# An attention, DFT and FFN kernel on one core: ScalarE's table load started early by a constant copy, filling work of PE as wide products, and the rounding of batch 1's y moved ahead of batch 0's last statistics

## Chip, cores and metric

The kernel runs on one core of one Trainium2 chip, as one launch. The metric is the device time in microseconds (us); the comparison is between medians of executions of the two kernels.

The engines are called PE (TensorE), DVE (VectorE), ACT (ScalarE), POOL (GpSimd) and SP (SyncE, which here only starts transfers). PEld are PE's weight loads.

## The reference, cut to what matters

```python
# attention: 2 batches, 8 heads, 768 rows, head width 64, all float32
mask = q_bucket[:, :, :, None] == k_bucket[:, :, None, :]   # buckets: signs of q @ proj and k @ proj, 6 bits
scores = np.where(mask, scale * q @ k.T, -1e9)
x = softmax(scores) @ v                    # -> (2, 768, 512)
# mixing and feed-forward
mixed = np.real(np.fft.fft(np.fft.fft(x, axis=1), axis=2))
u = x + mixed
un = (u - mean(u)) / np.sqrt(var(u) + 1e-6)              # per row
x = u + np.maximum(un @ w_ch1, 0) @ w_ch2                # 512 -> 2048 -> 512
# gated output
gate = sigmoid(causal depthwise convolution of x, 5 taps)
out = (gate * (x @ w_val)) @ w_out
```

## The kernel before, in words

Every engine has its own instruction list, written out by hand and run in order; semaphores (`wait_ge`, `then_inc`) are the only ties between the lists. So what stands ahead in an engine's list holds back what is behind it. A wide float32 product is made of three products of rounded values: each operand is split into a `_hi` part (rounded by ACT) and a `_lo` part (the rest, by DVE or POOL).

**Start.** SP and ACT issue the loads of the first head (`q_raw`, `k_raw`), `proj` and others. POOL sets the constants: it adds 1 to `consts_ready` for `minus_scale`, `w_q`, `w_k`, `zero`, `minus_half` and `ident`, and once more when `ident` holds the unit matrix. ACT then waits for `k_raw` and casts it to `k_a` (`round_k`, L701), casts `q_a` (L705) and copies `q_b` (L710). POOL makes `k_b` (L497) and the low half of `q_a` (L502). PE in the meantime makes the hash bits of q and k (L1299), DVE turns them into bits (L1000), PE into bucket numbers (L1305), and DVE writes the other halves of `q_b` and `k_b` (L1004, L1005). The first scores (L1346) need all four operands. Between these steps PE does filling work: `keep_busy(n)` makes n transposes of the unit matrix into bank 7, three times (17, 5 and 14), and nobody reads them. ACT's first computing instruction is the one of L701, and a table load is placed in front of it.

**Attention.** Eight pairs of heads run through 12 slots each: scores, row minimum (DVE L1012), exponential (ACT L718), transposes (L1413), product with v (L1363).

**DFT.** For each batch b the rows are folded, and PE forms y, the DFT along the sequence, in five banks: `sequence_step(b, t, blocks)` (L1386) adds step t to some of the blocks 0 to 4, and `seq_full` tells that a block is complete. ACT rounds each block to `y_hi` (L840), DVE takes the rest `y_lo` (L1170), and both copy a mirrored edge of the blocks 0 to 2 (L843, L1174). PE then does the DFT along the features in four steps per batch (`feature_dft`, L1494). Step 0 waits block by block for `y_lo`, step 1 for all mirrored edges.

**Statistics.** Each batch has six tiles of 128 rows; tile n of 0 to 5 is batch 0. For each: the sine bank is copied (ACT L816, `sine_part`), DVE forms cosine minus and plus sine (`cos_and_sin`, L1126), POOL and DVE add them to x (L630, L633, `mirrored_add` L1136), DVE takes the moments (L1090), the aggregate (L1094) and the sum with eps (L1098), POOL the inverse root `rstd` (L618), DVE the `shift` (L1104), ACT writes the normalised tile `un` (`normalise`, L807), PE transposes it (`transpose_un`, L1468), ACT rounds it (`unT_hi`, L799) and DVE takes the rest (`unT_lo`, L1112).

The loops of the two batches overlap. Before the change the order around the turn from batch 0 to batch 1 is:

- ACT: normalise of tile 3; five rounds of y of batch 1; three mirror copies; `unT_hi` of tile 3; normalise of tiles 4 and 5; then sine copies, with `unT_hi` of tiles 4 and 5 between.
- DVE: statistics of tiles 4 and 5 with their shifts; five `y_lo` of batch 1; three mirror copies; `unT_lo` of tile 3; cosine step; `unT_lo` of tile 4; cosine step; and so on.
- PE: the last step of the sequence DFT of batch 1, transpose of tile 3, features step 0, transpose 4, step 1, transpose 5, steps 2 and 3.
- POOL: the inverse root of tile 5 stands ahead of the first add of batch 1.

**FFN and output.** After features step 3 PE begins the FFN of batch 0: `ffn1` (L1549) waits for the cosine step of tile group 2 of batch 1 and for `unT_lo` of tile 5; `open_acc` (L1535) for the last cosine step. From there on the lists are long loops over 16 blocks of the FFN for each batch (L1549, L1563), and then the value and output products.

Of the kernel before, what the change touches and what calls it, by code (L numbers as in the profile page):

```python
# [6 lines left out]
def attention_fft_ffn_gate_kernel(nc, qT, kT, v, proj, w_ch1, w_ch2, w_val, conv_wT, w_out,  # L7
# [19 lines left out]
    P = 128  # L27
# [24 lines left out]
    with ctx:  # L52
# [632 lines left out]
        def _(act):  # L685
# [4 lines left out]

            def scale_first(h):

                act.wait_ge(qk_loaded[h], loads(0, h))
                act.mul(q_raw[h][:, :], q_raw[h][:, :], -SCALE).then_inc(q_scaled, 1)
# [137 lines left out]

            for b in range(B):
                for blk in range(5):
                    act.wait_ge(seq_full, 5 * b + blk + 1)

                    need(act, feat_full, 4 * b)
                    src = PS[:, SEQ_BANKS[b][blk], :]
                    size = HALF + 1 if blk < 3 else HALF
                    act.copy(y_hi[:, blk, 0:size], src[:, 0:size]).then_inc(y_hi_done, 1)  # L840
                for blk in range(3):
                    act.wait_ge(y_hi_done, 8 * b + blk + 1)
                    act.copy(y_hi[:, blk, HALF + 1:HALF + P], y_hi[:, blk, 1:P].bitcast(F32)).then_inc(y_hi_done, 1)  # L843
                if b:
                    unT_hi(T - 3)
                    normalise(T - 2)
                    normalise(T - 1)
                for t in range(T):
                    n = b * T + t
                    if t in (0, 2, 3):  # L850
                        sine_part(4 * b + t)
                    if b and t < 2:
                        unT_hi(T - 2 + t)
                    if not b and t >= LAG:
                        unT_hi(n - LAG)
                    if 2 <= t < (T - 1 if b else T):
                        normalise(n - 2)
                    if b and t == 3:
                        relu(0, 0)
# [112 lines left out]
        def _(dve):  # L972
# [190 lines left out]
            dve.wait_ge(fold_edge, 12)  # L1163
            for b in range(B):
                for blk in range(5):

                    dve.wait_ge(y_hi_done, 8 * b + blk + 1)
                    size = HALF + 1 if blk < 3 else HALF
                    src = PS[:, SEQ_BANKS[b][blk], :]
                    dve.tensor_tensor(y_lo[:, blk, 0:size], src[:, 0:size], y_hi[:, blk, 0:size].bitcast(F32),  # L1170
                                      ALU.subtract).then_inc(y_lo_done, 1)
                for blk in range(3):
                    dve.wait_ge(y_lo_done, 8 * b + blk + 1)
                    dve.tensor_copy(y_lo[:, blk, HALF + 1:HALF + P], y_lo[:, blk, 1:P].bitcast(F32))\  # L1174
                       .then_inc(y_lo_done, 1)
                if b:
                    unT_lo(T - 3)
                for t in range(T):
# [3 lines left out]
                    if t % 2:  # L1182
                        mirrored_add(n)
                    if t >= 2:
# [4 lines left out]
                    if b and t < 2:  # L1189
                        unT_lo(T - 2 + t)  # L1190
# [6 lines left out]
                moments(n)  # L1197
                aggregate(n)
                shift(n - 1)
                add_eps(n)  # L1200
                shift(n)
# [90 lines left out]
        def _(pe):  # L1292
# [151 lines left out]
            keep_busy(14)  # L1444
# [60 lines left out]
            for b in range(B):  # L1505
                if b:
# [234 lines left out]
```

## Time and profile before

| | |
|---|---|
| median of 3 runs | 635.16 us (634.46 to 636.32) |
| the profiled execution | 635.57 us |
| its span, first to last instruction | 633.9 us |
| mean granted clock of PE | 0.997 |
| instructions | 11055 |
| PE busy | 618.7 us, 98% |
| DVE busy | 346.1 us, 55% |
| ACT busy | 317.4 us, 50% |
| POOL busy | 250.7 us, 40% |
| DMA, mean over the span | 66 GB/s |

All times below are in microseconds from the start of the span, unless marked ns. A row of a timeline gives the start, how long the group lasted from the start of its first to the end of its last instruction, the engine, the line of the kernel, the operation, what it writes and reads, and how many instructions are merged (x5). In brackets stands how long the engine had been idle before, and what ended that. Successive instructions of one engine overlap a little, so the step from start to start is shorter than one's own duration. The granted clock is a share of PE's full 2.4 GHz: 1.00, or 0.50 for 1.2 GHz.

### The profile page before, as it was taken

To read this page: it belongs to the slowest core of one execution; us is meant where nothing else is said; L and a number is where in the kernel's file an instruction comes from. 1 tells how busy PE (TensorE), PEld (TensorE's weight loads), DVE (VectorE), ACT (ScalarE), POOL (GpSimd) and SP (SyncE) were. 2 spreads that over 40 slices of the span, in tenths; PEclk is the share of its full clock that TensorE was granted. 3 is DMA by queue.
4 is the path that set the end of the run, shared out by engine and by line. 5 is a ranking of instruction groups with operands and counts; after the bars stand their busy time and mean duration, and the time that the engine had idled before them with its cause. 6 is when DMAs were issued, how large, how long until landed. Compare 5 with 4: busy or idle time off the path is not lost.

```text
span 633.9 us, 11055 instructions
## 1 busy us (share of the span) xinstructions
PE 618.7 (98%) x3766; PEld 505.4 (80%) x3766; DVE 346.1 (55%) x587; ACT 317.4 (50%) x609; POOL 250.7 (40%) x213
## 2 busy tenths in 40 slices
PE   5899999999999999989999999999999999999998
PEld 4676777767777676989888888888888888888786
DVE  2888888887888875787111111117333333349820
ACT  3777777777777883464333222225233332444242
POOL 4533444333347664346333233327444434403140
PEclk9999999999999999999999999999999999999999
DMA  5762323223333020000211222620222221000202
GB/s 133 193 151 71 88 63 88 73 76 87 80 103 90 12 64 1 1 1 23 79 48 53 66 66 66 199 68 13 87 66 66 66 66 49 1 1 2 83 18 99
DMA packets 34267, 42.15 MB, mean 66 GB/s; under 512 B 3520, under 2 KB 22208, under 8 KB 34240
## 3 DMA queue, kind: packets, MB, share of 16 engines
q1 hardware_dynamic: 32272, 37.38, 20.6%
q0 software_dynamic: 1728, 4.02, 2.6%
q10 hardware_dynamic: 240, 0.39, 0.3%
q8 instruction: 17, 0.28, 0.2%
q14 instruction: 10, 0.08, 0.0%
HBM read 38.63 MB, written 3.15 MB: 66 GB/s over the span
## 4 chain that ended last, share of the span: by engine, by line
PE 90%; DVE 4%; ACT 2%; issue 2%; POOL 1%; DMA 1%; ACTq 0%; POOLq 0%; DVEq 0%
PE banks L1563 21%; PE banks L1549 21%; PE banks L1346 12%; PE banks L1363 11%; PE banks L1413 10%; PE banks L1642 5%; PE banks L1386 2%; PE banks L1494 2%; PE banks L1626 2%; PE banks L1299 2%; DVE x_then_u_then_gate L1213 1%; DMA k_raw<-in_k 1%; PE banks L1421 1%; PE banks L1305 1%; PE banks L1468 1%
## 5 line engine op out<-in xcount | busy, mean ns | idle before, releaser
L1143 DVE SCALAR_TENSOR_TENSOR h_lo<-banks,h_hi 128x512 fp32r<-128x512 f32 x64 | 35.4, 558 | 169.4 <-ACT h_hi L831 169.4
L1012 DVE TENSOR_REDUCE row_min<-banks 128x1 f32<-128x768 f32 x96 | 91.7, 956 | 33.9 <-PE banks L1346 33.4
L718 ACT ACTIVATE prob<-banks,row_min 128x768 f32<-128x768 f32 x96 | 87.0, 906 | 31.3 <-DVE row_min L1012 31.2
L1549 PE MATMUL banks<-unT_hi,w_hi 128*128 128x512 f32 (+1 forms) x256 | 86.4, 338 | 0.2 <-DVE h_lo L1143 0.2
L1549 PE MATMUL banks<-unT_hi,w_lo 128*128 128x512 f32 (+1 forms) x256 | 86.3, 337 | 0.0
L1549 PE MATMUL banks<-unT_lo,w_hi 128*128 128x512 f32 (+1 forms) x256 | 86.2, 337 | 0.0
L1413 PE MATMUL banks<-ident,prob 128*128 128x128 f32 x576 | 79.3, 273 | 1.3 <-ACT probT L350 1.3
L563 POOL TENSOR_TENSOR w_lo<-w_stage,w_hi 128x512 fp32r<-128x512 f32 x32 | 45.3, 1414 | 86.6 <-ACT w_hi L749 86.6
L1413 PEld LDWEIGHTS banks<-ident,prob 128*128 128x128 f32 x576 | 68.1, 140 | 6.7 <-issue 1.8
L831 ACT ACTIVATE h_hi<-banks 128x512 fp32r<-128x512 f32 x64 | 31.2, 490 | 79.4 <-PE banks L1549 79.3
L1363 PE MATMUL banks<-probT,v_in 128*64 128x384 f32 x384 | 69.0, 494 | 0.0
L568 POOL TENSOR_TENSOR w_lo<-w_stage,w_hi 128x512 fp32r<-128x512 f32 x32 | 42.2, 1317 | 67.2 <-ACT w_hi L754 67.2
L1563 PE MATMUL banks<-h_lo,w_hi 128*128 128x512 f32 (+1 forms) x256 | 66.0, 339 | 0.0
L1563 PE MATMUL banks<-h_hi,w_hi 128*128 128x512 f32 (+1 forms) x256 | 66.0, 339 | 0.0
L1563 PE MATMUL banks<-h_hi,w_lo 128*128 128x512 f32 (+1 forms) x256 | 65.6, 338 | 0.0
L754 ACT CAST w_hi<-w_stage 128x512 fp32r<-128x512 f32 x32 | 19.9, 621 | 88.6 <-PE banks L1563 88.6
L1213 DVE SCALAR_TENSOR_TENSOR x_then_u_then_gate<-x2T,taps,x_then_u_then_gate 128x384 f32<-128x384 f32 (+1 forms) x64 | 58.9, 926 | 4.9 <-DVE x_then_u_then_gate L1213 2.6
L1346 PE MATMUL banks<-k_a,q_a 128*128 128x384 f32 x192 | 57.6, 381 | 3.8 <-POOL q_a L502 2.8
L350 ACT COPY probT<-banks 128x384 f32<-128x384 f32 x104 | 49.0, 479 | 22.4 <-PE banks L1413 22.1
L497 POOL TENSOR_TENSOR k_b<-k_raw,k_a 64x768 fp32r<-64x768 f32 x16 | 29.2, 1826 | 72.1 <-ACT k_a L701 72.0
L1346 PEld LDWEIGHTS banks<-k_a,q_a 128*128 128x128 f32 x192 | 30.0, 191 | 32.6 <-issue 29.7
L1549 PEld LDWEIGHTS banks<-unT_hi,w_hi 128*128 128x128 f32 x256 | 48.1, 188 | 7.3 <-DVE h_lo L1143 0.4
(156 smaller groups left out, 1191.0 us busy)
## 6 DMA issues: line engine op xcount, KB each, us to landing
w_stage<-in_moe_w_ch SPq DMA_DIRECT2D x64, 256.0 KB, 2.8
q_raw<-in_q SPq DMA_DIRECT2D x32, 192.0 KB, 3.3
k_raw<-in_k SPq DMA_DIRECT2D x30, 192.0 KB, 3.6
v_in<-in_v SPq DMA_DIRECT2D x16, 192.0 KB, 2.8
out<-y_out SPq DMA_DIRECT2D x12, 256.0 KB, 2.0
seq_tables_sb<-in_dft POOLq DMA_DIRECT2D x6, 386.0 KB, 3.5
wvo_stage<-in_moe_w_val SPq DMA_DIRECT2D x1, 1024.0 KB, 5.7
wvo_stage<-in_moe_w_out SPq DMA_DIRECT2D x1, 1024.0 KB, 8.9
```

Of the source, the lines that this page charges most:

```text
L350: copy(dst, src).then_inc(scratch_free[bank_of(i, use)], 1)
L563: pool.tensor_tensor(w1_lo[:, slot, :, :], w1_stage[:, slot, :, :], w1_hi[:, slot, :, :].bitcast(F32), ALU.subtract).then_inc(w1_lo_done, 1)
L568: pool.tensor_tensor(w2_lo[:, slot, :], w2_stage[:, slot, :], w2_hi[:, slot, :].bitcast(F32), ALU.subtract).then_inc(w2_lo_done, 1)
L718: act.activation(prob[s % 2][:, :, :], s_tile(s), ACT.Exp, bias=row_min[:, s:s + 1], scale=-1.0, accum_out=row_sum[:, s:s + 1]).then_inc(e ...
L1012: dve.tensor_reduce(row_min[:, s:s + 1], s_tile(s), AX.XY, ALU.min).then_inc(min_ready, 1)
L1143: dve.scalar_tensor_tensor(out=h_lo[:, slot, at:at + size], in0=h_bank[c], scalar=0.0, in1=h_hi[:, slot, at:at + size].bitcast(F32), op0=A ...
L1213: dve.scalar_tensor_tensor(out=dst, in0=src, scalar=weight, in1=dst, op0=ALU.mult, op1=ALU.add).then_inc(conv_step, 1)
L1346: op = pe.matmul(s_tile(s)[:, c, :], lhs[:, rows], rhs[:, c * HALF:(c + 1) * HALF], start=start, stop=not start)
L1363: op = pe.matmul(PS[g * D:(g + 1) * D, 7, 0:HALF], v_in[:, h, kt, :], probT[h][:, kt, g * HALF:(g + 1) * HALF], start=(kt == 0), stop=(kt ...
L1413: op = pe.transpose(bank[:, j * P:(j + 1) * P], prob[tile % 2][:, c, j * P:(j + 1) * P], ident[:, :])
L1549: op = pe.matmul(h_bank[c], w_[:, slot, kb, :], x_[:, kb, at:at + size], start=(kb == 0 and m == 0), stop=(kb == KB - 1 and m == 2))
L1563: op = pe.matmul(acc(d, c), w_[:, slot, cols], h_[:, slot, at:at + size], start=False, stop=last, skip_group_check=True)
```

## The change

Three edits, on four engines.

1. ACT, after its DMA issues: a wait for `consts_ready` 5 and a copy of `zero` to one column of `row_sum`.
2. PE: `keep_busy` makes one float32 product of the unit matrix with several copies of itself, up to 384 columns (`blocks` of 128), where it made as many transposes as it was told: 3, 3 and 2 blocks in place of 17 transposes, 2 in place of 5, 3 and 3 in place of 14.
3. The order around the turn to batch 1. ACT: rounds 0 and 1 of y of batch 1 come ahead of the normalise of tile 3, which comes after round 2; the normalise of tile 4 after the mirror copies, that of tile 5 after the first sine copy and `unT_hi` of tile 3. DVE: `y_lo` 0 and 1 ahead of the shift of tile 4; the statistics of tile 5 after all `y_lo` and mirror copies; `unT_lo` of tile 3 after the first cosine step, with the shift of tile 5 behind it; `unT_lo` of tile 5 after the third cosine step. PE: the transposes of tiles 3, 4 and 5 each one features step later.

```diff
             act.dma_start(k_raw[0][D:2 * D, :], k_first).then_inc(qk_loaded[0], 16)
 
+            act.wait_ge(consts_ready, 5)
+            act.copy(row_sum[:, 0:1], zero[:, :])
...
             for b in range(B):
-                for blk in range(5):
-                    act.wait_ge(seq_full, 5 * b + blk + 1)
...
+                for blk in range(2 * b, 5):
+                    round_y(b, blk)
+                    if b and blk == 2:
+                        normalise(T - 3)
                 for blk in range(3):
-                    act.wait_ge(y_hi_done, 8 * b + blk + 1)
-                    act.copy(y_hi[:, blk, HALF + 1:HALF + P], y_hi[:, blk, 1:P].bitcast(F32)).then_inc(y_hi_done, 1)
+                    mirror_y(b, blk)
                 if b:
-                    unT_hi(T - 3)
                     normalise(T - 2)
-                    normalise(T - 1)
                 for t in range(T):
                     n = b * T + t
                     if t in (0, 2, 3):
                         sine_part(4 * b + t)
-                    if b and t < 2:
-                        unT_hi(T - 2 + t)
+                    if b and t < 3:
+                        unT_hi(T - 3 + t)
+                    if b and t == 0:
+                        normalise(T - 1)
                     if not b and t >= LAG:
                         unT_hi(n - LAG)
-                    if 2 <= t < (T - 1 if b else T):
+                    if 2 <= t < T - 1:
                         normalise(n - 2)
+                    if not b and t == T - 1:
+                        round_y(1, 0)
+                        round_y(1, 1)
...
             for b in range(B):
                 for blk in range(5):
...
+                    split_y(b, blk)
+                    if b and blk == 1:
+                        shift(T - 2)
                 for blk in range(3):
...
+                    mirror_y(b, blk)
                 if b:
-                    unT_lo(T - 3)
+                    moments(T - 1)
+                    aggregate(T - 1)
+                    add_eps(T - 1)
                 for t in range(T):
                     n = b * T + t
                     if t in (0, 1, 2, 4):
                         cos_and_sin(4 * b + STEP_OF[t])
                     if t % 2:
                         mirrored_add(n)
+                    if b and t == 0:
+                        unT_lo(T - 3)
+                        shift(T - 1)
+                    if b and t == 2:
+                        unT_lo(T - 1)
                     if t >= 2:
                         shift(n - 2)
                     if t >= 1:
                         moments(n - 1)
                         aggregate(n - 1)
-                    if b and t < 2:
-                        unT_lo(T - 2 + t)
+                    if b and t == 1:
+                        unT_lo(T - 2)
...
-                moments(n)
-                aggregate(n)
-                shift(n - 1)
-                add_eps(n)
-                shift(n)
+                if b:
+                    moments(n)
+                    aggregate(n)
+                    shift(n - 1)
+                    add_eps(n)
+                    shift(n)
...
-            def keep_busy(count):
-
-                for n in range(count):
-                    pe.transpose(PS[:, 7, 0:P], ident[:, :], ident[:, :])
+            def keep_busy(blocks):
+
+                pe.matmul(PS[:, 7, 0:blocks * P].rearrange("p (a m) -> p a m", a=blocks), ident[:, :],
+                          ident[:, :].unsqueeze(1).broadcast_to([P, blocks, P]), start=True, stop=True)
 
             pe.wait_ge(consts_ready, 7)
-            keep_busy(17)
+            for blocks in (3, 3, 2):
+                keep_busy(blocks)
             pe.wait_ge(w_ready, 2)
             prepare(-1, (0, "B"))
-            keep_busy(5)
+            keep_busy(2)
             pe.wait_ge(codes_loaded, 16)
             prepare(-1, (0, "C0"))
             prepare(-1, (0, "C1"))
-            keep_busy(14)
+            for blocks in (3, 3):
+                keep_busy(blocks)
...
                     transpose_un(2)
                     sequence_step(b, 2, range(1, 5))
-                    transpose_un(3)
                 for k in range(4):
                     feature_dft(4 * b + k)
-                    if b and k < 2:
-                        transpose_un(T - 2 + k)
+                    if b and k < 3:
+                        transpose_un(T - 3 + k)
```

`round_y`, `split_y` and the two `mirror_y` hold the instructions of the loops that they replace, unchanged.

## Rows read from the trace of the kernel before

**Rows 1.** The page, part 1: busy us, share of the span, instructions.

```profile
PE 618.7 (98%) x3766; PEld 505.4 (80%) x3766; DVE 346.1 (55%) x587; ACT 317.4 (50%) x609; POOL 250.7 (40%) x213
```

**Rows 2.** Chain of work that ended last, start: start us, us, what.

```profile
2.39 6.01 DMA k_raw<-in_k
8.47 1.28 ACT L701
9.77 0.84 ACT k_a L701
10.75 1.82 POOL k_b L497
12.71 1.81 POOL q_a L502
14.65 1.62 PE banks L1346 x4
16.27 1.44 PE banks L1299 x8
17.71 1.08 PE banks L1346 x4
...
26.95 0.98 PE banks L1346 x4
28.58 0.78 PE banks L1299 x8
```

**Rows 3.** Timeline of the start, 0 to 14 us.

```profile
2.39 0.62 ACTq L689 DMA_DIRECT2D k_raw<-in_k  x1
...
3.17 3.89 PE L1434 MATMUL banks<-ident 128*128 128x128 f32 x17 [3.17 <-POOL ident L482]
...
9.72 0.59 PE L1305 MATMUL banks<-bits_sb,bucket_codes_sb 128*128 128x384 f32 x2 [0.44 <-DVE bits_sb L1000]
...
10.15 1.69 PE L1434 MATMUL banks<-ident 128*128 128x128 f32 x14
...
12.08 0.62 DVE L1005 TENSOR_SCALAR k_b<-banks,bucket_ones_sb 64x384 fp32r<-64x384 f32 x1
```

**Rows 4.** Busy us by engine in three stretches; PEclk is the granted clock.

```profile
core 0: us, PE busy (x) PEld busy (x) DVE busy (x) ACT busy (x) POOL busy (x), PEclk, DMA share, GB/s
11.84:14.62 2.78, 0.00 (x0) 0.00 (x0) 0.85 (x2) 1.83 (x3) 2.56 (x3) 1.00 0.00 0
14.62:18.03 3.41, 3.38 (x13) 1.73 (x14) 1.21 (x2) 0.73 (x1) 1.78 (x1) 0.50 0.09 14
...
276.73:278.44 1.71, 0.00 (x1) 0.03 (x1) 1.05 (x6) 1.71 (x7) 0.55 (x1) 1.00 0.00 0
```

**Rows 5.** Timeline of the middle, 275 to 287 us.

```profile
275.38 1.99 ACT L840 CAST y_hi<-banks 128x385 fp32r<-128x385 f32 x5
...
275.86 0.68 DVE L1090 BATCH_NORM_STATS2 stats<-x_then_u_then_gate 128x6 f32<-128x512 f32 x1
...
277.61 0.21 DVE L1104 TENSOR_SCALAR minus_mean_times_rstd<-mean_var,rstd 128x1 f32<-128x1 f32 x1 [0.66 <-POOL rstd L618]
277.74 2.41 DVE L1170 TENSOR_TENSOR y_lo<-banks,y_hi 128x385 fp32r<-128x385 f32 x5
...
278.44 0.36 PE L1494 MATMUL banks<-feat_cos_hi_sb,y_hi 128*128 128x258 f32 x1 [1.71 <-DVE y_lo L1170]
...
280.07 0.49 DVE L1174 CAST y_lo<-y_lo 128x127 fp32r<-128x127 f32 x3
...
280.67 0.60 PE L1468 MATMUL banks<-ident,un 128*128 128x128 f32 x4
280.87 0.38 ACT L816 COPY sin_part<-banks 128x256 f32<-128x256 f32 x1 [1.01 <-PE banks L1494]
...
281.33 0.76 DVE L1126 TENSOR_TENSOR cos_minus_plus_sin<-banks,sin_part 128x257 f32<-128x257 f32 x2 [0.18 <-issue]
...
285.93 0.21 DVE L1104 TENSOR_SCALAR minus_mean_times_rstd<-mean_var,rstd 128x1 f32<-128x1 f32 x1
...
286.24 0.39 PE L1549 MATMUL banks<-unT_hi,w_hi 128*128 128x512 f32 x1
```

**Rows 6.** Line L1136 of DVE, its six adds: ns min/median/max.

```profile
L1136 DVE TENSOR_TENSOR x_then_u_then_gate<-x_then_u_then_gate,cos_minus_plus_sin x6: 416/494/926, 262.8 to 292.0; 128x255 f32<-128x255 f32 x6
```

More of the change, by code:

```diff
@@ L831, in relu, with round_y, mirror_y @@
                     act.activation(h_hi[:, slot, at:at + size], h_bank[c], ACT.Relu).then_inc(h_hi_done, 1)
-            for b in range(B):
-                for blk in range(5):
-                    act.wait_ge(seq_full, 5 * b + blk + 1)
[L837 to L840, printed above, removed]
+            def round_y(b, blk):
+                act.wait_ge(seq_full, 5 * b + blk + 1)
+                need(act, feat_full, 4 * b)
+                src = PS[:, SEQ_BANKS[b][blk], :]
+                size = HALF + 1 if blk < 3 else HALF
+                act.copy(y_hi[:, blk, 0:size], src[:, 0:size]).then_inc(y_hi_done, 1)
+            def mirror_y(b, blk):
+                act.wait_ge(y_hi_done, 8 * b + blk + 1)
+                act.copy(y_hi[:, blk, HALF + 1:HALF + P], y_hi[:, blk, 1:P].bitcast(F32)).then_inc(y_hi_done, 1)
+            for b in range(B):
+                for blk in range(2 * b, 5):
+                    round_y(b, blk)
+                    if b and blk == 2:
+                        normalise(T - 3)
                 for blk in range(3):
-                    act.wait_ge(y_hi_done, 8 * b + blk + 1)
-                    act.copy(y_hi[:, blk, HALF + 1:HALF + P], y_hi[:, blk, 1:P].bitcast(F32)).then_inc(y_hi_done, 1)
+                    mirror_y(b, blk)
                 if b:
-                    unT_hi(T - 3)
                     normalise(T - 2)
-                    normalise(T - 1)
                 for t in range(T):
@@ L1163, in _, with split_y, mirror_y @@
             dve.wait_ge(fold_edge, 12)
+            def split_y(b, blk):
+                dve.wait_ge(y_hi_done, 8 * b + blk + 1)
+                size = HALF + 1 if blk < 3 else HALF
+                src = PS[:, SEQ_BANKS[b][blk], :]
+                dve.tensor_tensor(y_lo[:, blk, 0:size], src[:, 0:size], y_hi[:, blk, 0:size].bitcast(F32),
+                                  ALU.subtract).then_inc(y_lo_done, 1)
+            def mirror_y(b, blk):
+                dve.wait_ge(y_lo_done, 8 * b + blk + 1)
+                dve.tensor_copy(y_lo[:, blk, HALF + 1:HALF + P], y_lo[:, blk, 1:P].bitcast(F32))\
+                   .then_inc(y_lo_done, 1)
             for b in range(B):
                 for blk in range(5):
[L1167 to L1171, printed above, removed]
+                    split_y(b, blk)
+                    if b and blk == 1:
+                        shift(T - 2)
                 for blk in range(3):
-                    dve.wait_ge(y_lo_done, 8 * b + blk + 1)
-                    dve.tensor_copy(y_lo[:, blk, HALF + 1:HALF + P], y_lo[:, blk, 1:P].bitcast(F32))\
-                       .then_inc(y_lo_done, 1)
+                    mirror_y(b, blk)
                 if b:
-                    unT_lo(T - 3)
+                    moments(T - 1)
+                    aggregate(T - 1)
+                    add_eps(T - 1)
                 for t in range(T):
```

## The prediction, made blind

> **What bounds the kernel now.** The page's busy shares first: TensorE (PE) is busy 98% of the span [rows 1]. With such a share, an edit gains only where PE stands still or runs slowly, so I looked for those places, first in the chain of work that ended last, then in the timeline of the two stretches that the change touches.
>
> The first is the start. Up to 14.65 us the chain is not on PE [rows 2]: the k_raw load lands at 8.40 (2.39 + 6.01), ScalarE's table load takes 1.28, its cast of k_a 0.84, two GpSimd subtractions 1.82 and 1.81, and only then come the first scores. PE does nothing from 11.84 to 14.62; its granted clock, 1.00 until then, fell there, was 0.50 (1.2 GHz) for 3.41 us and full (2.4 GHz) again from 18.03 [rows 4].
>
> The second is the middle. PE is idle for 1.71 us before the feature DFT of batch 1 at 278.44, waiting for y_lo [rows 5]. VectorE began its five y_lo pieces only at 277.74, and its own queue had held them: the last shift of batch 0 stands ahead, and that had waited 0.66 for GpSimd's rstd [rows 5]. The data was long there: ScalarE's rounds of y began at 275.38. After 278.44 PE works without a gap into the FFN (L1549, from 286.24) and on to the end, so what is won before the FFN is won whole.
>
> **Part 1, the table load.** The constant copy waits for five of GpSimd's settings; PE's first fill, which waits for all seven, began at 3.17, and ScalarE's last DMA issue ends at 3.01 [rows 3]. So the load runs from 3.2 at the latest to 4.5, and even at the 0.38 of a sine copy of 256 columns (this one has one [rows 5]) the copy is done by 4.9. Queued behind the wait is only the k_a cast, whose data lands at 8.40: 3.5 us of cover. The cast then starts at 8.48, not 9.77, and q_a on GpSimd ends at 13.24. VectorE's k_b, also needed by the scores, ends at 12.70 (12.08 + 0.62 [rows 3]) and is not moved; it becomes the next-latest with half a microsecond to spare. Scores at 13.37: **gain 1.28**. Bounds: 0 if the load stays where it is, else 1.28.
>
> The Trainium skill ("ScalarE: Activation LUTs", What ACT_TABLE_LOAD costs) gives about 1.28 us for the load and another 1.38 of drain; the sum by it would be 1.4 larger. The trace shows the 1.28 and the cast directly behind it, so the measurement decides.
>
> **Part 2, the fill.** 17, 5 and 14 transposes become 8, 2 and 6 blocks, in products of up to 384 columns. The trace has no such product; the nearest are the bit products, four of 384 columns side by side in 0.78 at the full clock and 1.44 at half [rows 2]. A three-block product costs at most that. First fill, at half rate (229 ns for each of its 17 transposes, 121 for the later 14 [rows 3]): 8/3 x 1.44 = 3.8, to 7.0; before, it ended at 7.06. Second: 0.5 to 1.0, ahead of the bucket products at 9.72, which wait for bits_sb. Third: 1.6 to 2.9 from 10.15, ended by 11.7 to 13.1, still before 13.37. So the fill costs nothing in itself.
>
> What it may change is the clock: PE's idle time before the scores goes from 2.78 to 1.7 (13.37 - 11.7), between 0.3 and 1.9. An idle time of 1.71 in the middle left the clock at 1.00 [rows 4]. The half clock cost, in the chain: scores 1.62 where a like group takes 0.98, bits 1.44 for 0.78, scores 1.08 for 0.98 [rows 2]: 0.64 + 0.66 + 0.10 = **1.40**. I take it as gone, for the row of 1.71 is the nearest; bounds 0 and 1.40, and below zero in rival D.
>
> **Part 3, the rests of y.** On ScalarE two rounds of batch 1 go ahead of the normalise of the fourth tile. That normalise ended just before 275.38 and takes 0.72 from start to start, so the rounds can begin at 274.66; at 1.99/5 = 0.4 each [rows 5] three end by 275.9, and the other two, behind the normalise, at 277.0 and 277.3. VectorE was free at 275.86, where the last statistics of batch 0 began [rows 5]. Now it does there y_lo 0 and 1 (2.41/5, 0.47 from start to start), the shift of the fifth tile at 276.8, and y_lo 2 to 4, done at 278.35. The mirror casts (0.4) and the statistics of tile 5 (0.68 and 0.35 for aggregate and eps) follow, and the first cosine step stands at 279.76.
>
> PE's last work before its wait was transpose 3, ended at 276.73; without it PE is free at 276.3. It starts on y_lo 0 at 276.5 and is then paced by the pieces: features of step 0 issued by 278.87 and transpose 3 by 279.3, where both were done at 281.03 less the 0.36 of the next transpose, 280.67 [rows 5]. That is **1.4 for PE alone**, the upper bound.
>
> But the FFN needs VectorE's last unT_lo of batch 0, and VectorE is now the tighter queue. From its first cosine step to the end of the step before the FFN it took from 281.33 to 285.93, 4.60 for nine pieces of work [rows 5]. Now the same pieces, a shift (0.13) and the last unT_lo, which comes behind them (0.68), follow 279.76: 279.76 + 4.60 + 0.13 + 0.68 = 285.17. I followed the waits inside: the sine copy comes at 279.45, GpSimd's rstd of tile 5 at 280.4, ahead of batch 1's first add on its queue, whose parts come at 280.5; ScalarE's normalise of tile 5, behind which its unT_hi waits, at 282.05; PE's transpose 5 at 283.15 and its unT_hi at 283.8. None is late. FFN at 285.25 instead of 286.24: **gain 0.96**, with PE idle for about 0.5 ahead of it. Lower bound 0, if VectorE stretches: its mirrored add takes from 0.42 to 0.93 [rows 6], the long one beside a GpSimd add, and two such stretches eat the gain. Behind the FFN's start PE next waits for the last cosine step, which would come at about 289.2; PE gets there at 289.4: no stall, little spare.
>
> The Trainium skill ("SBUF — State Buffer", Who interferes with whom) says that a VectorE instruction with two SBUF inputs contends with a GpSimd instruction that reads SBUF. The 0.42 and 0.93 agree; by it the sum would lose up to 0.5 if the add of tile 7 meets a GpSimd add.
>
> **Sum.** The profiled execution took 635.57 (span 633.9, and 1.67 around it), 0.41 above the median of 635.16. From it: 635.57 - 1.28 - 1.40 - 0.96 = 631.93. The runs shown spread from 634.46 to 636.32, a little more than the clock term; the lowest, taken as one without the fall, gives 634.46 - 2.24 = 632.2. I forecast **632.1**.
>
> **Rivals.**
> A, the clock still falls. For it: 1.7 of idle may be 1.9, and the work around it differs from that in the middle. Against it: 1.71 in the middle left the clock full. Time 635.57 - 2.24 = 633.3.
> B, the middle gives nothing: VectorE's queue, already 0.5 behind PE, is stretched by another 1.0 by GpSimd or by an order of waits that I misread. Time 631.93 + 0.96 = 632.9, and 634.3 with the clock fall.
> C, the table load does not go: it is placed elsewhere, or a second appears before the exponentials. For it: the trace cannot show where a load for such a copy is put. Against: the load before was brought on by a cast of ScalarE and served the exponentials too. Time 631.93 + 1.28 = 633.2, and 634.6 with the fall.
> D, slower: the wide products hold the clock up less than the transposes do, as they put a third of the instructions and weight loads on PE. Then the early bit and bucket products run at half (k_b later by about 0.9, past q_a by 0.4) and the half clock lasts two more stretches like the one of 3.41, each costing at most 1.7: 635.57 - 2.24 + 0.4 + 3.4 = 637.1. It decides only if the half clock outlasts the first scores by over 5 us. Against it: the first fill keeps PE as long as before (3.8 for 3.89).
> The Trainium skill ("TensorE: Matmul & The Clock Gate", What's actually happening) says that the half rate is the default and that activity releases it; the transposes of the first fill at 229 ns and of the third at 121 agree, and nothing here shows what a wide product counts.
>
> **How the numbers follow.** Chances: forecast 0.50, A 0.25, B 0.14, C 0.07, D 0.04. The forecast's own range is 631.0 to 633.0 (middle term 0.5 to 1.4, run to run 0.5); A, and B and C with the fall, take it to 634.5; low end 630.9. A measurement of this kernel can tell 0.3%, 1.9 us, from no change, so below 633.25 is faster. The forecast lies below, as do B and C without the fall; A lies on the line and is split. Faster 0.70, within 0.26, slower 0.04.
>
> **What would show it.** The table load near 3.0 and the k_a cast near 8.5; scores near 13.4; granted clock 1.00 behind them; PE's idle time before the features of batch 1 near 0.2 in place of 1.71, and a new one of 0.5 before the first L1549 matmul, ended by unT_lo. The forecast is wrong if k_b ends the wait for the first scores, if the clock still reads 0.50 behind them, or if PE waits for the last cosine step before it opens the accumulators.

## The result, and the profile after

| | median of runs | ratio to before, 95% interval |
|---|---|---|
| before, in the same session | 634.15 us (633.31 to 636.32) | |
| changed kernel | 631.18 us (630.56 to 632.11) | 0.9945 [0.9931, 0.9959] |

The kernel became 0.55% faster (0.41% to 0.69%), which is 2.6 to 4.4 us. The forecast was a gain of 3.06 us and a time of 632.1 in the range 630.9 to 634.5. The two medians differ by 2.97 (ratio 0.9953), inside that interval. The gain is confirmed, but the level came out lower: the ratio times the median beside it is 630.7, below the low end of the range, and the median of the changed kernel, 631.18, lies only just inside it. The last sections say why.

First the page of the changed kernel: its span, and its part 1 (busy us, share of the span, instructions), against [rows 1].

```profile
span 629.7 us, 11008 instructions
PE 619.7 (98%) x3742; PEld 503.0 (80%) x3742; DVE 345.8 (55%) x587; ACT 317.8 (50%) x610; POOL 250.8 (40%) x213
```

The span went from 633.9 to 629.7, 4.2 us. PE has 24 instructions fewer (the filling work) and ScalarE one more (the copy); the shares have not moved. So the gain is again to be looked for in the places where PE stood still.

Start, ScalarE, then PE: timeline of the changed kernel (start us, us, engine, line, operation, out<-in, count, and in brackets the idle time before and what ended it). These answer [rows 2, 3].

```profile
2.76 1.28 ACT L692 ACT_TABLE_LOAD   x1 [2.76 <-issue]
4.06 0.19 ACT L692 COPY row_sum<-zero 128x1 f32<-128x1 f32 x1
7.92 0.83 ACT L704 CAST k_a<-k_raw 128x768 fp32r<-128x768 f32 x1 [3.68 <-DMA q_raw<-in_q]
```
```profile
3.17 3.78 PE L1466 MATMUL banks<-ident 128*128 128x384 f32 x6 [3.17 <-POOL ident L482]
...
8.32 1.22 PE L1466 MATMUL banks<-ident 128*128 128x256 f32 x2
9.23 0.98 PE L1338 MATMUL banks<-bits_sb,bucket_codes_sb 128*128 128x384 f32 x2
10.01 2.77 PE L1466 MATMUL banks<-ident 128*128 128x384 f32 x4
12.82 0.59 PE L1379 MATMUL banks<-k_a,q_a 128*128 128x384 f32 x2
```

The table load has left the path: it runs at 2.76, long before the first head's data has landed, and the cast stands at 7.92 with no load ahead of it. The data released ScalarE at 8.47 before and at 7.92 here, which is a difference of landing, not of the kernels; what belongs to the kernel is the distance from there to the first scores: 14.65 - 8.47 = 6.18 before, 12.82 - 7.92 = 4.90 now. It is 1.28 shorter, the length of the load. The scores took 0.59 for their first pair where they took 0.98 at the half clock: no fall of the clock here. The products ahead of them were still at the half rate in this execution: the third filling took 2.77 (1.45 at the full rate, in wide_only below) and so reached up to the scores.

The chain of work that ended last, in the changed kernel (start us, us, what), against the chains of [rows 2].

```profile
12.82 0.97 PE banks L1379 x4
...
29.52 2.09 PE banks L1396 x12
...
262.42 3.19 PE banks L1419 x18
...
272.74 0.47 DVE y_lo L1185
273.22 0.14 issue
273.35 2.51 PE banks L1529 x15
275.86 0.44 PE banks L1503 x4
276.30 1.08 PE banks L1529 x9
277.38 0.44 PE banks L1503 x4
277.82 1.79 PE banks L1529 x15
279.61 0.44 PE banks L1503 x4
280.04 1.81 PE banks L1529 x15
281.85 0.18 issue
282.04 4.43 PE banks L1583 x24
286.47 2.62 PE banks L1569 x24
```

And four rows of the same chain in the kernel before, the points to measure from:

```profile
32.76 2.09 PE banks L1363 x12
...
265.62 3.19 PE banks L1386 x18
...
286.40 4.23 PE banks L1549 x24
290.63 1.42 PE banks L1535 x13
```

Read point by point: at the first product with V the changed kernel is 3.24 ahead (32.76 to 29.52), at the sequence products of the middle 3.20 (265.62 to 262.42), at the accumulators 4.16 (290.63 to 286.47), at the end 4.2. So all of it arises in two places, 3.2 in the start and 0.96 in the middle, and nothing is given back behind them. The 3.24 of the start is 0.55 of landing (8.47 to 7.92), 1.28 of table load, and 1.41 behind the first scores, which is the half clock of [rows 2, 4].

Middle, VectorE, against [rows 5]: timeline of the changed kernel.

```profile
272.66 1.01 DVE L1185 TENSOR_TENSOR y_lo<-banks,y_hi 128x385 fp32r<-128x385 f32 x2
273.59 0.20 DVE L1120 TENSOR_SCALAR minus_mean_times_rstd<-mean_var,rstd 128x1 f32<-128x1 f32 x1
273.71 1.48 DVE L1185 TENSOR_TENSOR y_lo<-banks,y_hi 128x385 fp32r<-128x385 f32 x3
...
281.25 0.68 DVE L1128 TENSOR_TENSOR unT_lo<-banks,unT_hi 128x512 fp32r<-128x512 f32 x1
...
285.08 0.76 DVE L1142 TENSOR_TENSOR cos_minus_plus_sin<-banks,sin_part 128x257 f32<-128x257 f32 x2
```

What PE waited for in 262 to 300 us (us in total, times, longest), changed kernel:

```profile
PE banks L1529 <- DVE y_lo L1185: 0.3, 1, 0.3
PE banks L1583 <- issue: 0.2, 1, 0.2
```

The wait of 1.71 is down to 0.3. The one in front of the FFN (L1583) is put down to "issue"; VectorE's last unT_lo ended at 281.93 and the FFN began at 282.04, so I read it as the unT_lo that ended it; moments_late, below, bears this out.

### The profile page after: what moved, and what is told of

It is laid out like the page before. It is cut to its first block, busy times and chain, and to the rows that moved or that the text cites. A ratio compares the mean times of both kernels' runs of the same rounds, so it can differ in the third digit from the quotient of the medians.

```text
span 629.7 us, 11008 instructions
## 1 busy us (share of the span) xinstructions
PE 619.7 (98%) x3742; PEld 503.0 (80%) x3742; DVE 345.8 (55%) x587; ACT 317.8 (50%) x610; POOL 250.8 (40%) x213
## 4 chain that ended last, share of the span: by engine, by line
PE 91%; DVE 4%; ACT 2%; issue 1%; POOL 1%; ACTq 0%; POOLq 0%; DVEq 0%
PE banks L1597 21%; PE banks L1583 21%; PE banks L1379 12%; PE banks L1396 11%; PE banks L1446 10%; PE banks L1676 5%; PE banks L1419 2%; PE banks L1529 2%; PE banks L1660 2%; PE banks L1332 2%; DVE x_then_u_then_gate L1246 1%; PE banks L1466 1%; PE banks L1338 1%; PE banks L1454 1%; PE banks L1503 1%
## 5 line engine op out<-in xcount | busy, mean ns | idle before, releaser
L1583 PE MATMUL banks<-unT_hi,w_hi 128*128 128x512 f32 (+1 forms) x256 | 86.6, 338 | 0.4 <-issue 0.2
L1583 PE MATMUL banks<-unT_hi,w_lo 128*128 128x512 f32 (+1 forms) x256 | 86.4, 337 | 0.0
L1583 PE MATMUL banks<-unT_lo,w_hi 128*128 128x512 f32 (+1 forms) x256 | 86.3, 337 | 0.0
L1583 PEld LDWEIGHTS banks<-unT_hi,w_hi 128*128 128x128 f32 x256 | 48.1, 188 | 7.6 <-DVE h_lo L1159 0.4
```

The lines of the kernel that those rows point to most:

```text
L1583: op = pe.matmul(h_bank[c], w_[:, slot, kb, :], x_[:, kb, at:at + size], start=(kb == 0 and m == 0), stop=(kb == KB - 1 and m == 2))
```

## The experiments

All ran with their own executions of the kernel before beside them on the same chip, in three groups, each on another chip: copy_only, wide_only, y_only and no_wide (median of the kernel before 634.61 us); no_y, no_copy, after_again and no_third (634.98); moments_late, long_third, no_fill and no_wide_again (634.91). Of two kernels of different groups the ratios are compared, not the times. In what follows a *fallen* execution is one whose mean granted clock over the span is below 0.9985: one stretch like the 3.41 us at 0.50 of [rows 4] lowers a mean over 634 us by 0.0027. This counts only what the record of the clock shows; the last section says what it misses. Of the executions of the kernel before, 63 of 81 are fallen.

### One part alone

**copy_only**: the kernel before, with the copy.

```diff
+            act.wait_ge(consts_ready, 5)
+            act.copy(row_sum[:, 0:1], zero[:, :])
```

> The kernel before with the constant copy alone (fill by transposes, old order of y). Theory 1 (each part gives its own term): the load runs near 3 us, the k_a cast starts right after its data, first scores 1.28 us earlier relative to the landing of k_raw, and the clock term stays with the wide fill: gain 1.3 us over the kernel before. Theory 2 (the clock term belongs to the shorter idle time of PE, whatever fills it): with the idle time at 1.5 us the clock doesn't fall any more, gain 1.3 plus what the fall costs in the runs of before that have it, about 1.7 to 2.5 us.

Measured: 632.79 us, ratio 0.9973 [0.9962, 0.9985]; 3 of 12 executions fallen. Its timeline of PE in the start:

```profile
9.40 1.69 PE L1437 MATMUL banks<-ident 128*128 128x128 f32 x14
12.65 0.58 PE L1349 MATMUL banks<-k_a,q_a 128*128 128x384 f32 x2 [1.56 <-POOL q_a L502]
13.07 0.51 PE L1349 MATMUL banks<-k_b,q_b 128*128 128x384 f32 x2
```

The k_a cast stands at 7.74, so the scores come 4.91 behind it, as in the changed kernel. And with the old transposes as filling work the clock is full behind the scores: the idle time ahead of them is 1.56 in place of 2.82. The copy brings its own term and the shorter idle with it.

**wide_only**: the kernel before, with the wide products.

```diff
-                for n in range(count):
-                    pe.transpose(PS[:, 7, 0:P], ident[:, :], ident[:, :])
+                pe.matmul(PS[:, 7, 0:blocks * P].rearrange("p (a m) -> p a m", a=blocks), ident[:, :],
+                          ident[:, :].unsqueeze(1).broadcast_to([P, blocks, P]), start=True, stop=True)
...
-            keep_busy(17)
+            for blocks in (3, 3, 2):
+                keep_busy(blocks)
...
```

> The kernel before with the wide filling products alone. Theory 1: no end of the chain moves, the clock stays up behind them: gain 0.4 to 1.4 us. Theory 2: PE still idles for 2.5 us or more before the first scores, so nothing changes: 0 +- 0.5 us. Theory 3 (the wide products count less for the clock than the transposes, as the profile after has them at the half rate up to 12.8 us): the clock is at half for a stretch that reaches into the first scores in most runs: 0.5 to 1.5 us slower.

Measured: 634.76 us, ratio 1.0001 [0.9985, 1.0016]; 11 of 12 fallen. PE's timeline:

```profile
9.69 1.45 PE L1433 MATMUL banks<-ident 128*128 128x384 f32 x4
14.19 0.59 PE L1346 MATMUL banks<-k_a,q_a 128*128 128x384 f32 x2 [3.05 <-POOL q_a L502]
14.62 0.59 PE L1346 MATMUL banks<-k_b,q_b 128*128 128x384 f32 x2
15.14 0.85 PE L1299 MATMUL banks<-q_raw,w_q 128*32 128x384 f32 x2
```

The third filling took 1.45 against 1.69, so PE stood idle longer, 3.05, and the bit products behind the first scores took 0.85 a pair where the full clock gives 0.52 (13.51 in copy_only): the clock fell. Wide products alone gain nothing that these executions can tell: the interval is 1.0 us to either side, and a gain of the whole 1.40 (ratio 0.9978) lies outside it.

**y_only**: the kernel before, with the order of y of the change (on ScalarE and VectorE, and PE's transposes of tiles 3, 4 and 5), of which the core is

```diff
+                    if not b and t == T - 1:
+                        round_y(1, 0)
+                        round_y(1, 1)
...
+                    split_y(b, blk)
+                    if b and blk == 1:
+                        shift(T - 2)
```

> The kernel before with the new order of y alone. Theory 1: PE's wait before the features of batch 1 goes from 1.71 to about 0.2 us, a new one of 0.5 or less stands before the first FFN product, and the accumulators open 0.96 us earlier: gain 1.0 us. Rival: the gain is taken back behind the FFN's start, gain below 0.5 us.

Measured: 632.94 us, ratio 0.9977 [0.9965, 0.999]. From the x18 row of its chain to the accumulators it is 289.82 - 265.74 = 24.08, against 290.63 - 265.62 = 25.01 before: 0.93 gained, in the middle alone. In the start nothing changed (6.19 from the load to the scores, idle 2.83, the clock fell in its profile and was at 0.50 from 13.7 to 20.5, 6.8 us). Only 4 of 12 executions are fallen, though, which the new order can't explain, and the ratio is better by it.

### One part undone

**no_wide**: the changed kernel with the 17, 5 and 14 transposes of before.

```diff
...
-            for blocks in (3, 3, 2):
-                keep_busy(blocks)
+            keep_busy(17)
...
-            keep_busy(2)
+            keep_busy(5)
...
-            for blocks in (3, 3):
-                keep_busy(blocks)
+            keep_busy(14)
```

> The kernel after with the fill by transposes as before (copy and order of y stay). Theory 1: it loses the clock term, 0.4 to 1.4 us slower than the kernel after, gain over before 2.2 us. Theory 2 (the shorter idle time does it): as fast as the kernel after, 3 to 3.5 us under before. Theory 3 (wide products hold the clock less): up to 0.5 us faster than the kernel after.

Measured: 631.11 us, ratio 0.9944 [0.9926, 0.9961]; none of 6 fallen. **no_wide_again**, the same kernel in another group:

> The kernel no_wide (copy and order of y, fill by transposes) once more beside the others, since it had half as many executions as the rest. If wide products and transposes are worth the same: 0.994 to 0.996 of the kernel before, as the kernel after.

Measured: 631.44 us, 0.9938 [0.9917, 0.996]; none of 6 fallen. With transposes the changed kernel is, within the intervals, as fast as with wide products (0.9945). In PE's timeline of no_wide the idle time is 1.56 and the clock stays:

```profile
9.54 1.69 PE L1467 MATMUL banks<-ident 128*128 128x128 f32 x14
12.80 0.58 PE L1379 MATMUL banks<-k_a,q_a 128*128 128x384 f32 x2 [1.56 <-POOL q_a L502]
```

**no_copy**: the changed kernel without the two lines of the copy.

```diff
-            act.wait_ge(consts_ready, 5)
-            act.copy(row_sum[:, 0:1], zero[:, :])
```

> The kernel after without the constant copy (wide fill and order of y stay). Theory 1: 1.3 us slower than the kernel after. Theory 2 (PE's longer idle time before the first scores lets the clock fall): 1.3 us plus the fall in most runs, 2 to 2.7 us slower, with a mean granted clock of 0.997 or less in most of its executions.

Measured: 633.78 us, 0.9974 [0.9959, 0.9989]; 7 of 12 fallen. The load stands at 7.75 again, the scores 6.18 behind it, after an idle time of 2.93, with the clock down behind them, in spite of the wide products. It is 2.1 slower than the changed kernel beside it (below).

**no_y**: the changed kernel with the old order of y (all of edit 3 undone; two places of it shown).

```diff
-                    if b and blk == 1:
-                        shift(T - 2)
...
-                    if not b and t == T - 1:
-                        round_y(1, 0)
-                        round_y(1, 1)
```

> The kernel after with the old order of y (copy and wide fill stay). If the middle is worth its 0.96 us of the sum: 0.8 to 1.1 us slower than the kernel after, run beside it. Rival (the timed runs give y more than the trace does, since copy_only to no_wide differed by 1.7): 1.5 us or more slower than the kernel after.

Measured: 632.36 us, 0.9965 [0.9953, 0.9977]. The old wait is back; what PE waited for in 262 to 300 us:

```profile
PE banks L1499 <- DVE y_lo L1173: 1.7, 1, 1.7
```

From the x18 row to the accumulators 287.10 - 262.10 = 25.00. The granted clock stayed at 1.00 behind these 1.73 us of idle time, as in [rows 4].

**after_again**: the changed kernel in this group.

> The kernel after once more, beside these three. By the sum without any clock term 2.24 us under before, by what was measured 3.0 to 3.5 us under it. In executions whose mean granted clock is 1.00 on both sides the difference should be 2.2 to 2.4 us; the rest is the share of executions in which the clock falls: most of before's, less than a third of its own.

Measured: 631.67 us, 0.9953 [0.9938, 0.9968]; 2 of 9 fallen. Beside it no_y, of which 6 of 12 are fallen, is 0.69 slower, a little under the 0.8 to 1.1 expected.

### The filling work

**no_third**: the changed kernel without the third filling (it leaves out only products that nobody reads).

```diff
-            for blocks in (3, 3):
-                keep_busy(blocks)
```

> The kernel after with the third filling (two products of 384 columns) left out. If the idle time of PE is what lowers the clock: PE is idle for 2.8 us or more before the scores again, as in before, and most executions show 0.997 or less, 0.8 to 1.2 us slower than the kernel after. If the filling after the bucket products doesn't matter for the clock: as fast as the kernel after.

Measured: 633.03 us, 0.9977 [0.9965, 0.9988], 1.36 slower than the changed kernel beside it; 7 of 12 fallen. PE's timeline:

```profile
9.19 0.58 PE L1338 MATMUL banks<-bits_sb,bucket_codes_sb 128*128 128x384 f32 x2 [0.60 <-DVE bits_sb L1016]
12.85 0.98 PE L1379 MATMUL banks<-k_a,q_a 128*128 128x384 f32 x2 [3.08 <-POOL q_a L502]
13.62 0.84 PE L1379 MATMUL banks<-k_b,q_b 128*128 128x384 f32 x2
```

The scores come as early as ever (4.89 behind the cast) but run at the half rate after 3.08 of idle time: a long idle stretch, with the copy in place, brings the fall back in this profile. The clock did not wait for the end of that stretch: the record has it at 0.50 from 10.8 to 17.6, so from 1.1 us after PE's last product. And the five executions that don't count as fallen have a median of 633.19, no better than the seven that do (632.92); how that can be, no_fill shows.

**no_fill**: the changed kernel with no filling at all (it leaves out only those products).

```diff
-            for blocks in (3, 3, 2):
-                keep_busy(blocks)
...
-            keep_busy(2)
...
-            for blocks in (3, 3):
-                keep_busy(blocks)
```

> The kernel after with no filling work at all. The hash-bit and bucket products run at the half clock, so VectorE's k_b ends about 0.9 us later and past q_a (k_b takes over the wait for the first scores, by up to 0.5 us), and the first scores, bits and the slots behind them run at half until the clock rises: 1.5 to 3 us slower than the kernel after. If filling work is not worth its place: less than 0.5 us slower.

Measured: 633.29 us, 0.9972 [0.9959, 0.9984]. PE's timeline: bits, buckets and scores all at the half rate, until 17.5.

```profile
7.03 0.85 PE L1332 MATMUL banks<-q_raw,w_q 64*32 64x384 f32 x2 [7.03 <-DVE q_raw L996]
...
9.38 0.98 PE L1338 MATMUL banks<-bits_sb,bucket_codes_sb 128*128 128x384 f32 x2 [0.85 <-DVE bits_sb L1016]
13.03 0.98 PE L1379 MATMUL banks<-k_a,q_a 128*128 128x384 f32 x2 [2.67 <-POOL q_a L502]
```

The mean granted clock of all twelve executions reads 0.999 or 1.000, though products run at the half rate: the record of the clock doesn't show a half rate that stands from the start. The scores are 4.89 behind the cast all the same: even with buckets at the half rate VectorE's k_b, ended at 12.60, doesn't take over from q_a, ended at 12.88, though it had been expected to. By the ratios it is some 1.2 to 1.7 us slower than the changed kernel (0.9953 and 0.9945), so the filling work as such is worth having.

**long_third**: no_wide with 22 transposes in the third filling in place of 14.

```diff
-            keep_busy(14)
+            keep_busy(22)
```

> The kernel no_wide (copy, order of y, fill by transposes) with 22 transposes in the third filling in place of 14, so that PE's idle time before the first scores is about 0.6 us in place of 1.56. If a shorter idle time still matters for the clock: 0.2 to 0.5 us under no_wide and the kernel after. If the clock is already held by the shorter idle time that the copy brings: the same within 0.3 us. Where the clock is at half during this filling it would end behind q_a: up to 1 us slower.

Measured: 631.62 us, 0.994 [0.9918, 0.9962]; none of 6 fallen. In its profile the clock rose late, the filling took 3.54 and held the scores back to 13.49, 5.38 behind the cast instead of 4.90. More filling than the gap holds buys nothing measurable.

### The spare of the middle

**moments_late**: the changed kernel with VectorE's statistics of tiles 6 and 7 of batch 1 moved behind the last unT_lo.

```diff
+                    if b and t == 2:
+                        moments(n - 2)
+                        aggregate(n - 2)
+                        add_eps(n - 2)
+                        moments(n - 1)
+                        aggregate(n - 1)
+                        add_eps(n - 1)
...
-                    if t >= 1:
+                    if t >= 1 and not (b and t < 3):
```

> The kernel after with the statistics of batch 1's first tile (moments, aggregate, eps) moved on VectorE from ahead of the last two unT_lo of batch 0 to behind them. If VectorE's queue is what holds the FFN's start in the kernel after: the short wait before the first L1549 product goes, the accumulators open 0.2 to 0.4 us earlier relative to the first step of the features, and the time is 0.2 to 0.4 us lower. If PE's own work bounds it: the same place. If the last cosine step is now late (it has 0.4 us to spare): a wait before the accumulators and no gain.

Measured: 632.37 us, 0.9956 [0.994, 0.9971]. What PE waited for in 262 to 300 us:

```profile
PE banks L1576 <- DVE cos_minus_plus_sin L1142: 1.2, 1, 1.2
PE banks L1536 <- DVE y_lo L1185: 0.3, 1, 0.3
```

The small wait ahead of the FFN is gone, so VectorE's queue was what held it, and a longer one stands in front of the accumulators, for the last cosine step. From x18 to the accumulators 288.18 - 263.31 = 24.87, 0.82 more than in the changed kernel. Its start shows one more thing. Scores at 12.79 after 1.79 of idle time, and the fall 1.2 us behind it; busy us by engine in two stretches, with the granted clock (PEclk) after the busy columns:

```profile
11.00:12.79 1.79, 0.00 (x0) 0.03 (x1) 1.09 (x2) 1.47 (x2) 1.72 (x2) 1.00 0.01 3
...
14.00:18.00 4.00, 4.00 (x21) 3.15 (x14) 2.55 (x4) 1.53 (x3) 0.53 (x1) 0.57 0.70 190
```

### The runs side by side

Idle time of PE ahead of the first scores and the clock behind them are from the one profile of each kernel; fallen counts its timed executions. no_fill is left out, since its half rate is not in the record.

| kernel | copy | filling | idle ahead of scores, us | fall in the profile | fallen |
|---|---|---|---|---|---|
| before | no | transposes | 2.82 | yes | 63 of 81 |
| wide_only | no | wide | 3.05 | yes | 11 of 12 |
| y_only | no | transposes | 2.83 | yes | 4 of 12 |
| no_copy | no | wide | 2.93 | yes | 7 of 12 |
| no_third | yes | wide, two of three | 3.08 | yes | 7 of 12 |
| moments_late | yes | wide | 1.79 | yes | 4 of 9 |
| copy_only | yes | transposes | 1.56 | no | 3 of 12 |
| no_wide, both | yes | transposes | 1.56 | no | 0 of 12 |
| no_y | yes | wide | 1.45 | no | 6 of 12 |
| after_again, after | yes | wide | 0.40, none | no | 4 of 16 |
| long_third | yes | 22 transposes last | none | no | 0 of 6 |

With 2.8 us of idle time or more 92 of 129 executions are fallen, with less than 1.8 it is 17 of 67. Of those 67, the ones with transposes count 3 of 30 and the ones with wide products 14 of 37. What a fall costs: the kernel before has a median of 633.47 without and 634.80 with it in the first group (8 and 19 executions), 633.65 and 635.06 in the second (7 and 20), 633.80 and 634.91 in the third (3 and 14), so 1.1 to 1.4. The fallen ones here are those with a mean clock of 0.996 or 0.997, one fall; two, five and three more have a lower mean. In the changed kernels the difference is less, 0.4 in no_y and in moments_late.

## Why the prediction was right or wrong

**What bounds the kernel.** Right. PE is the bound, and the two places named are those from which the whole difference comes.

**Part 1, 1.28.** Right, to the hundredth. From ScalarE's first instruction behind the landing to the first scores it is 6.18, 6.17, 6.19 and 6.18 in the four profiles without the copy and 4.89 to 4.92 in nine with it (long_third, whose filling holds the scores, apart). The load ran at 2.76, where "from 3.2 at the latest" was forecast, and a copy of a constant served the casts and the exponentials too: no second load stands ahead of the exponentials (the one other load, L906 here and L890 before, is in both kernels), so rival C is out. k_b ended at 12.46 and q_a at 12.67: 0.2 to spare instead of 0.5, as bits and buckets ran at the half rate in this execution; it did not decide even in no_fill. The Trainium skill ("ScalarE: Activation LUTs", What ACT_TABLE_LOAD costs) adds a drain of 1.38 us to the load's 1.28. The trace agrees with the 1.28 only: the copy begins 0.02 us behind the load, and the scores moved by 1.28, not by 2.66. The later load shows no drain either: it starts at 548.22, and ScalarE's next instruction at 549.51.

**Part 2, 1.40.** Right in size for an execution that had the fall and lost it (1.41 between the two profiles; 1.1 to 1.4 between the medians), and wrong in two steps.
- The first is where the term was put. It stands in the part on the filling work, and the sum of the parts reads as if the wide products were worth 1.40. No run shows a gain from them: 1.0001 alone, and 0.9944 and 0.9938 without them against 0.9945 and 0.9953 with them. It is the copy that makes the fall rarer: 3 of 12 with it alone and 0 of 12 in no_wide, against 63 of 81 before. It brings the scores 1.28 earlier and so cuts the idle time ahead of them; that the idle time is the way by which it acts is what no_third speaks for and y_only against. The prediction had both in its own figures (idle 2.78 to 1.7, of which 1.28 is the copy) and didn't separate them.
- The second is the step "I take it as gone, for the row of 1.71 is the nearest". A stretch of 1.73 in the middle of no_y left the clock at 1.00, and 1.79 ahead of the scores of moments_late was followed by a fall; and the changed kernel still has the fall in 4 of 16 executions, as rival A had it for all. The fall is a matter of shares, about three quarters before (63 of 81) and a quarter after. So by an estimate the term is worth 1.40 times the difference of the shares, some 0.7 in the mean over many executions. The copy's worth in medians agrees: 1.82 (before to copy_only), 1.83 (y_only to no_wide) and 2.1 (no_copy to the changed kernel), which is 1.28 and 0.5 to 0.8 more. It is no proof: between the executions without a fall alone the same three pairs differ by 0.72, 1.62 and 0.81, so the timed runs carry the 1.28 itself only to about half a microsecond, and the traces are what shows it.
- One reading under it was not safe either: the prediction has the granted clock at "1.00 until then" and in the next part the first fill at the half rate, 229 ns for each transpose. Both stand in the trace. In all fourteen profiles the record of the clock begins at 1.00, whatever the durations say, so at the start it is no evidence of the full rate.

The fill's own times: the first was forecast at 3.8 and took 3.78; the third at 1.6 to 2.9 and took 1.45 to 2.77. Rival D, that wide products hold the clock up less, named a weak effect of the right sign at most (14 of 37 fallen against 3 of 30, and in the changed kernel's profile the half rate lasted until 12.8) but not its consequence: nothing was lost that a median shows.

**Part 3, 0.96.** Right: 25.01 and 25.00 with the old order, 24.05 and 24.08 with the new one, so 0.93 to 0.96; rival B is out. (The prediction's own times, 286.24 and 285.25, differ by 0.99; it took 0.96.) The steps inside were near. The features began 10.93 behind the x18 row, where they were 12.82 behind it before: 1.89 earlier, forecast 1.94. Of that the transpose that moved behind takes 0.44. Ahead of the FFN PE stood idle for 0.18, where 0.5 was forecast: PE came later than I had it, since the y_lo pieces paced the first feature step (2.51 for 2.40). The FFN began 1.00 earlier against the x18 row (20.62 to 19.62), and 0.96 of it arrived at the accumulators. "Little spare" for the last cosine step was right too: in moments_late it became the wait, and cost 0.82. In medians this part shows as 0.69 (after_again against no_y) and as 1.67 and 1.68 (y_only, and copy_only to no_wide); the latter two pairs also differ in fallen executions, 63 of 81 to 4 of 12 and 3 of 12 to 0 of 6, so the traces are the better measure.

**The base, the step that failed.** The forecast of 632.1 stands between two sums, and each started too high. The first, 631.93, starts from one profiled execution of 635.57. Its fall is taken off by the 1.40, but its first data had also landed late: ScalarE was released at 8.47, where the thirteen other profiles have 7.62 to 8.63 with a median of 7.96, and no term takes off that half microsecond. The second is the step "the lowest, taken as one without the fall, gives 634.46 - 2.24 = 632.2". The 18 executions of the kernel before that have no fall took 633.17 to 633.98, so 634.46 was in all likelihood one with the fall (its own clock is not on record), and 2.24 off an execution without it, 633.47, is 631.2. The kernel before has medians of 634.15, 634.61, 634.98 and 634.91 with 7, 29, 32 and 20 executions. Had I started there, in the first group, an execution without the fall gives 633.47 - 1.28 - 0.96 = 631.2, one with it 634.80 - 1.28 - 1.40 - 0.96 = 631.2; 631.18 was measured. That this agrees to a few hundredths is luck in part, for the group ran apart from the result. Taken for one execution the terms were right, and the level was 0.9 high, and with a low end of 630.9 the range left no room for a base that is off by one microsecond, while the highest and the lowest of the three runs shown lay 1.9 apart.

**What stays open.** Why y_only had only 4 of 12 fallen with an idle time of 2.83, and no_y 6 of 12 with 1.45: the idle time ahead of the scores is not all that decides it. Nor does the fall keep to the end of the idle stretch: it came 1.1 us into it in no_third, at its end before (14.62), and 1.2 us behind it in moments_late. Why the clock rose late in some profiles with wide products (the changed kernel, after_again) and in one with transposes (long_third). That the wide products are behind the 14 of 37 is suggested by the counts, not shown: the groups ran at different times and on different chips, and the count misses a half rate that stands from the start.

## What to carry to other kernels

A table load that stands on ScalarE in front of the first data can be drawn forward by a copy of a constant, and is worth its full length, here 1.28, where that cast opens the chain; check that what was second in line (here k_b) has its own spare. Where two edits act on one idle stretch, give the clock's term to the one that changes the stretch, and count it by shares of executions, since a fall that the profile shows need not be in the median. Before a forecast of a few microseconds is set against a median, compare the landing of the first load in the profiled execution with others, and let the range be at least as wide as the runs of the base lie apart.

## What the runs showed of the hardware

- The granted clock of the profile doesn't tell the first rate of an execution. In no_fill the bits took 0.85 for a pair of products and the scores 0.98 where the full rate has 0.49 and 0.58, from the first product until 17.5 us, and its mean clock over the span reads 1.000. Early in a kernel the durations have to be read instead. For the same reason a count of fallen executions by the mean clock misses slow ones, all twelve of no_fill, and it seems the five of no_third.
- After one and the same filling of 3.78 us the bits ran at either rate: 0.76 then 0.49 in no_third, 0.85 throughout in the changed kernel. With the half rate still there the third filling of wide products took 2.77 instead of 1.45, and so covered the idle stretch by being slow.
- For filling work, products of 384 columns and transposes of 128 gave the same time of the kernel, within 1 us (ratio 1.0001 [0.9985, 1.0016]). The Trainium skill ("TensorE: Matmul & The Clock Gate", What's actually happening) says that activity releases the half rate; the rows of the changed kernel agree in the direction (without the third filling the scores ran at 0.98, with it at 0.59); in the kernel before they ran at 0.98 in spite of a third filling.
- The landing of the first load moved by 1.0 us (7.62 to 8.63) between profiles of kernels whose lists issue it alike. Up to 0.29 of that is the issue of its last part, which starts at 2.11 to 2.40. The 1.0 is as much as the whole gain of the middle, and it is in every time.
